# Retrieval from the memory in linear attention: one plain fp32 product against three split fp32r products, with feature map and memory each in a high and a low part

## The reference, cut to what matters

```python
B, H, S, D = 2, 8, 576, 64
scores = scale * q @ k.T ; causal mask ; a = softmax(scores)
local = a @ v
phi(x) = where(x > 0, x, exp(x) - 1) + 1
mem_ret = einsum('bhsd,bhde->bhse', phi(q), M_prev)          # the retrieval
mem_norm = einsum('bhsd,bhd->bhs', phi(q), z_prev) + 1e-6
out = g * mem_ret / mem_norm + (1 - g) * local               # g = sigmoid(beta), one per head
x = moe(out) ; result = moe2(x)
```

## Time and profile before

| | |
|---|---|
| median of 3 runs | 1149.52 us (1149.25 to 1149.59) |
| the profiled execution | 1149.53 us, its span 1147.7 us |
| TensorE busy | 1121.0 us (98%), 6932 matmuls |
| VectorE busy | 725.2 us (63%) |
| ScalarE busy | 513.6 us (45%) |
| GpSimd busy | 437.2 us (38%) |
| granted TensorE clock, mean | 0.997 of full speed |

### The profile page before, as it was taken

How to read it: one execution, slowest core, us unless ns; L and a number is a source line. 1 busy time by engine, 2 the same in 40 slices (tenths; PEclk the granted TensorE clock), 3 DMA queues, 4 the chain that set the end, 5 groups by cost and what they waited for, 6 DMA issues and landing times.

```text
span 1147.7 us, 21730 instructions
## 1 busy us (share of the span) xinstructions
PE 1121.0 (98%) x6932; PEld 1010.8 (88%) x6932; DVE 725.2 (63%) x1464; ACT 513.6 (45%) x1182; POOL 437.2 (38%) x506
## 2 busy tenths in 40 slices
PE   5999999999999999999999999999999999999998
PEld 3777779999999788898988989899999998998997
DVE  5888965345346877756566565675656656666564
ACT  4787867567567432443333333233332333323331
POOL 4778740000032442524425244352443433534331
PEclk8999999999999999999999999999999999999999
DMA  4513112002001101111111110111201111011002
GB/s 107 174 40 68 35 74 74 0 0 74 1 0 38 38 19 56 39 48 45 36 55 55 37 55 18 55 55 37 55 18 55 55 37 55 18 55 56 19 6 78
DMA packets 62128, 52.78 MB, mean 46 GB/s; under 512 B 32257, under 2 KB 49665, under 8 KB 62081
## 3 DMA queue, kind: packets, MB, share of 16 engines
q1 hardware_dynamic: 62080, 52.20, 14.9%
HBM read 49.83 MB, written 2.36 MB: 45 GB/s over the span
## 4 chain that ended last, share of the span: by engine, by line
PE 89%; DVE 4%; issue 3%; POOL 1%; ACT 1%; SPq 1%; DMA 0%; DVEq 0%; POOLq 0%; ACTq 0%
PE ps_y L1412 39%; PE ps_h L1412 26%; PE ps_g L1412 17%; PE ps_o L1412 2%; PE ps_s L1412 1%; PE ps_p L1441 1%; POOL prob L525 1%; PE ps_o L1453 1%; DVE zl L1181 1%; PE ps_y L1630 1%; DVE negmax L1031 0%; DMA beta_all<-in_beta_dram 0%; DVE nrm L1010 0%; DVE nrm_e L1014 0%; DVE ptl L974 0%
## 5 line engine op out<-in xcount | busy, mean ns | idle before, releaser
L832 ACT ACTIVATE zh<-h 128x256 fp32r<-128x256 f32 (+1 forms) x256 | 112.5, 445 | 332.5 <-POOL h L596 133.3
L1412 PE MATMUL ps_y<-w2c_h,zh 128*128 128x512 f32 x512 | 202.3, 395 | 0.2 <-DVE zl L1181 0.2
L1412 PE MATMUL ps_y<-w2c_l,zh 128*128 128x512 f32 x512 | 201.9, 394 | 0.0
L1412 PE MATMUL ps_y<-w2c_h,zl 128*128 128x512 f32 x512 | 199.3, 389 | 0.0
L591 POOL TENSOR_TENSOR h<-u,p 128x256 f32<-128x256 f32 (+1 forms) x64 | 57.0, 890 | 354.6 <-DVE u L1158 354.6
L1181 DVE SCALAR_TENSOR_TENSOR zl<-h,zh 128x256 fp32r<-128x256 f32 (+1 forms) x256 | 171.1, 673 | 7.2 <-ACT zh L832 6.6
L1412 PEld LDWEIGHTS ps_y<-w2c_h,zl 128*128 128x128 f32 x512 | 96.2, 188 | 21.9
L1412 PEld LDWEIGHTS ps_y<-w2c_h,zh 128*128 128x128 f32 x512 | 96.6, 189 | 13.9 <-DVE zl L1181 0.4
L1412 PEld LDWEIGHTS ps_y<-w2c_l,zh 128*128 128x128 f32 x512 | 96.6, 189 | 11.8
L1308 DVE SCALAR_TENSOR_TENSOR acc<-ps_y,weight,acc 128x512 f32<-128x512 f32 x112 | 82.1, 742 | 37.2 <-PE ps_y L1412 37.2
L596 POOL TENSOR_TENSOR h<-h,p 128x256 f32<-128x256 f32 (+1 forms) x64 | 61.0, 954 | 100.8 <-DVE h L1169 100.8
(11 more groups left out here) (212 smaller groups left out, 3086.2 us busy)
## 6 DMA issues: line engine op xcount, KB each, us to landing
rc<-in_moe_w_dram SPq DMA_DIRECT2D x64, 512.0 KB, 3.8
raw<-in_moe_w_in_dram SPq DMA_DIRECT2D x2, 2048.0 KB, 8.4
raw<-in_moe_w_out_dram SPq DMA_DIRECT2D x2, 2048.0 KB, 11.3
out_dram<-acc SPq DMA_DIRECT2D x9, 256.0 KB, 2.0
q_nat<-in_q_dram SPq DMA_DIRECT2D x16, 128.0 KB, 2.5
k_nat<-in_k_dram SPq DMA_DIRECT2D x16, 128.0 KB, 2.4
v_nat<-in_v_dram SPq DMA_DIRECT2D x16, 128.0 KB, 2.4
z_nat<-in_z_prev_dram SPq DMA_DIRECT2D x8, 64.0 KB, 3.0
```

The source lines that it names most:

```text
L832: act.activation(z_place(u, quarter, 0), rows, ACT.Relu).then_inc(e_hi, 1)
L1412: last = pe.matmul(dst, a[x], b[y], start=start and i == 0, stop=stop and i == 2)
```

## The change

The feature map of a pair is kept as `qph` and `qpl` and its memory as `mem_h` and `mem_l`, and the retrieval of each group becomes three split products. GpSimd makes `mem_l` at the start of the second part of `split_v`. VectorE makes `qpl` in `prep_lo`, now for items 3 and 4 too, in the loop at the steps `("item", 3)` and `("item", 4)`, and for pair 0 just ahead of the loop. ScalarE's copies go on as before, but release VectorE (`t_hi`) and no longer TensorE; `t_lo` is counted up by VectorE alone.

```diff
@@ -115,7 +115,8 @@
         vh, o = at_("vh", o, [P, 2, NJ, P], F32R)
         vl, o = at_("vl", o, [P, 2, NJ, P], F32R)
         mem_nat, o = at_("mem_nat", o, [P, P])
-        mem_t, o = at_("mem_t", o, [P, 2, P])
+        mem_h, o = at_("mem_h", o, [P, 2, P], F32R)
+        mem_l, o = at_("mem_l", o, [P, 2, P], F32R)
         z_nat, o = at_("z_nat", o, [P, P])
         phi_e, o = at_("phi_e", o, [P, NJ, P])
         phi_w, o = at_("phi_w", o, [P, NJ, P])
@@ -123,7 +124,8 @@
         qbl, o = at_("qbl", o, [P, 2, NQ, 2, QB], F32R)
         kh, o = at_("kh", o, [P, 2, S], F32R)
         kl, o = at_("kl", o, [P, 2, S], F32R)
-        qp, o = at_("qp", o, [P, 2, S])
+        qph, o = at_("qph", o, [P, 2, S], F32R)
+        qpl, o = at_("qpl", o, [P, 2, S], F32R)
         prob, o = at_("prob", o, [P, POFF[NQ]])
         pth, ptl = [], []
         for g in range(G):
@@ -386,7 +388,7 @@
                     sp.wait_ge(phi_exp, pair + 1)
                     sp.wait_ge(phi_relu, pair + 1)
                     load_heads(q_nat, q3, pair, ld_q)
-                    sp.wait_ge(v_split, 3 * pair + 3)
+                    sp.wait_ge(v_split, 4 * pair + 4)
                 else:
                     sp.wait_ge(nat_zeroed, 1)
                 load_heads(v_nat, v3, pair, ld_v)
@@ -448,7 +450,7 @@
         def _(pool):
             pool.sem_inc(phi_z, 1)
             pool.sem_inc(phi_q, 1)
-            pool.sem_inc(v_split, 3)
+            pool.sem_inc(v_split, 4)
             pool.sem_inc(s_eps, 9)
             pool.sem_inc(s_norm, 9)
 
@@ -504,10 +506,12 @@
                     settled()
                     pool.tensor_scalar(vh[:, half, :, :], v_nat[:, :, :], 1.0, 0.0, ALU.mult, ALU.add)\
                         .then_inc(v_split, 1)
-                    pool.tensor_scalar(mem_t[:, half, :], mem_nat[:, :], 1.0, 0.0, ALU.mult, ALU.add)\
+                    pool.tensor_scalar(mem_h[:, half, :], mem_nat[:, :], 1.0, 0.0, ALU.mult, ALU.add)\
                         .then_inc(v_split, 1)
                 else:
-                    pool.wait_ge(v_split, 3 * pair + 3 + 1)
+                    pool.wait_ge(v_split, 4 * pair + 4 + 2)
+                    pool.tensor_tensor(mem_l[:, half, :], mem_nat[:, :], mem_h[:, half, :].bitcast(F32),
+                                       ALU.subtract).then_inc(v_split, 1)
                     pool.tensor_tensor(vl[:, half, :, :], v_nat[:, :, :], vh[:, half, :, :].bitcast(F32),
                                        ALU.subtract).then_inc(v_split, 1)
 
@@ -631,7 +635,7 @@
         @block.scalar
         def _(act):
             act.preload_act_table_set("natural_log_exp_and_others")
-            act.sem_inc(t_hi, 3)
+            act.sem_inc(t_hi, 5)
             act.sem_inc(phi_exp, 1)
             act.sem_inc(phi_relu, 1)
             act.sem_inc(s_exp, 9)
@@ -658,10 +662,10 @@
                     last = copy(kh[:, half, NT * P:S], bank[:, P:P + TAIL])
                 elif item == 3:
                     act.wait_ge(o_ready, 3 * pair + 3)
-                    last = copy(qp[:, half, 0:NT * P], bank[:, :])
+                    last = copy(qph[:, half, 0:NT * P], bank[:, :])
                 else:
-                    last = copy(qp[:, half, NT * P:S], bank[:, 0:TAIL])
-                last.then_inc(t_hi if item < 3 else t_lo, 1)
+                    last = copy(qph[:, half, NT * P:S], bank[:, 0:TAIL])
+                last.then_inc(t_hi, 1)
 
             def phi(pair):
                 act.wait_ge(ld_q, 48 * pair + 48)
@@ -975,7 +979,7 @@
 
             def prep_lo(item, pair, half):
                 bank = prep_bank(item, pair)
-                dve.wait_ge(t_hi, 3 * pair + item + 4)
+                dve.wait_ge(t_hi, 5 * pair + item + 6)
                 rows_of = lambda h: slice(h * D, (h + 1) * D)
                 if item == 0:
                     for h in range(2):
@@ -985,6 +989,10 @@
                             scalar=SCALE, in1=qbh[r, half, 0:NQ - 1, h, :].bitcast(F32), op0=ALU.mult, op1=ALU.subtract)
                 elif item == 1:
                     last = less(kl[:, half, 0:NT * P], bank[:, :], kh[:, half, 0:NT * P])
+                elif item == 3:
+                    last = less(qpl[:, half, 0:NT * P], bank[:, :], qph[:, half, 0:NT * P])
+                elif item == 4:
+                    last = less(qpl[:, half, NT * P:S], bank[:, 0:TAIL], qph[:, half, NT * P:S])
                 else:
                     for h in range(2):
                         r = rows_of(h)
@@ -1065,7 +1073,7 @@
                     elif what == "x":
                         for group in group_at(t, pair, half, first):
                             x_lo(*group)
-                    elif what == "item" and more and t < 3:
+                    elif what == "item" and more:
                         prep_lo(t, pair + 1, 1 - half)
                     elif what == "phi" and more and t in (1, 3):
                         phi(t, pair + 1, 1 - half)
@@ -1092,6 +1100,8 @@
             row_sum(0, 0, 0)
             row_sum(1, 0, 0)
             dve.wait_ge(zeroed, 1)
+            for item in range(3, 5):
+                prep_lo(item, 0, 0)
             pairs(dve, body)
             probs_lo(NQ - 1, NP - 1, 1)
             x_lo(G - 2, NP - 1, 1)
@@ -1447,12 +1457,12 @@
 
                 pe.wait_ge(o_lo, 3 * pair + g + 3)
                 pe.wait_ge(t_lo, 5 * pair + 10)
-                pe.wait_ge(v_split, 3 * pair + 6)
+                pe.wait_ge(v_split, 4 * pair + 8)
                 cols = slice(3 * QB * g, 3 * QB * (g + 1))
 
-                pe.matmul(ps_o[:, 0:3 * P], mem_t[:, half, :],
-                          qp[:, half, cols].rearrange("p (b c) -> p b c", b=3).unsqueeze(2)
-                          .to_broadcast([P, 3, 2, QB]), start=True, stop=False)
+                products(ps_o[:, 0:3 * P], (mem_h[:, half, :], mem_l[:, half, :]),
+                         [x[:, half, cols].rearrange("p (b c) -> p b c", b=3).unsqueeze(2)
+                          .to_broadcast([P, 3, 2, QB]) for x in (qph, qpl)], True, False)
 
             def values(j, g, pair, half):
 
```

## The result

The changed kernel takes 1158.12 us (median of 6 runs, 1157.88 to 1158.84), the kernel before 1149.45 us on the same chip (6 runs, 1149.25 to 1149.84): a ratio of 1.0077 with an interval of 1.0064 to 1.009, so +8.7 us where +6.7 was forecast. It is slower, and the time lies within the range. The profiled execution took 1158.64 us (span 1156.7), 9.1 us more than the one of before; 0.4 us of this is not in the medians.

The account below looks back on a forecast made before the run. A ring of waits through the normalizer, with no engine full, was taken as the bound. 0.73 + 7 x (0.43 + 0.59 - 0.12) - 0.36 = +6.67 us gave 1156.2 us, range 1151.2 to 1160.

Parts of the forecast that it names:

- the range: Whole kernel: 1151.2 to 1160 us, the forecast's own part being 1154.5 to 1159.5.
- The bound and the sign: Attention loop: no engine is full, waits bound it; slower by over 0.2% was given 84%.
- the ring: Attention loop: waits closing once per 18.47 us period, two nearly equal legs, by TensorE and by ScalarE and GpSimd, through the normalizer.
- `mem_l`: GpSimd ahead of `vl`: 0.46 us long, delaying the normalizer through the end of `vl`; +0.43 us, 7 times.
- the sum: All terms: 0.73 + 7 x (0.43 + 0.59 - 0.12) - 0.36 = +6.67 us.
- The wait at item 4: TensorE's last feature-map transpose waits for VectorE's 512-column `qpl`, behind block 8's reciprocal: +0.59 us per pair.
- The retrieval: TensorE: three split products take 0.52 us against 0.65; 0.12 us less, counted once per pair in the loop.
- Block 8 behind the last `qpl`: TensorE's block 8 transposes wait for VectorE's last 64 columns; these just hide, by 0.06 us, so 0.
- Ahead of the loop: Pair 0's preparation: item 4 waits for VectorE's subtraction and the hop, +0.73 us once.
- The last three retrievals: After the last pair's preparation all three retrievals count: -0.36 us.
- TensorE itself carries the chain: After the last pair's preparation TensorE's own work was taken as the bound, so the last three retrievals count.

Follow-up runs that it names:

- e1: Kernel before with the retrieval as three fp32r products of the high parts alone, no low parts made; 1148.77 us, ratio 0.9996.
- e4: Changed kernel with GpSimd's `mem_l` moved behind `vl`; 1155.68 us, ratio 1.0054.
- e3: e1 plus the feature map's low part made by VectorE, which releases the banks; memory's low part left out; 1154.89 us, ratio 1.0046.
- e7: e4 with item 4's transpose behind the first value products of group 1 and block 8's transposes behind all of them; 1155.10 us, ratio 1.005.
- e6: Changed kernel with the moves of both e4 and e5; 1153.36 us, ratio 1.0036.
- e10: e7 plus the move of e5; 1155.41 us, ratio 1.005.
- e2: e1 plus the memory's low part made by GpSimd ahead of `vl`; feature map's low part left out; 1151.81 us, ratio 1.0022.
- e5: Changed kernel with VectorE's 512-column `qpl` of item 3 moved ahead of the reciprocal of block 8; 1155.69 us, ratio 1.0057.
- e9: Kernel before with only `vl` moved behind `prob` of block 8; 1152.08 us, ratio 1.0022.

## Why the prediction was right, and what was mis-sized

**The bound and the sign: right.** That a loss on either leg of the ring passes on whole is shown by the parts: 0.42 and 0.74 us a period by themselves, 1.15 together (18.43 in e1, 19.58 in the changed kernel, means of pairs 2 to 5).

**`mem_l`: right.** 0.46 us long as forecast, and 0.42 passes on against the 0.43 of the sum. e4 shows that it does so by the end of `vl`. The first pair pays as well, but by another way than the forecast's. There VectorE's normalizer is done ahead of `vl` (`nrm_g` at 32.41 + 0.17, `vl` at 32.51), and `phi_w` waits only for its turn in GpSimd's own queue: from the start of `vh` to that of `phi_w` it is 3.68 us (30.74, 34.42), 3.28 before (30.13, 33.41) and 3.28 in e3. So `mem_l` costs 0.40 there, and counting it seven times came out right.

**The wait at item 4: right in kind, 0.10 too small.** 0.59 was forecast; from the end of `prob` of block 7 to item 4 it is 0.69 longer. The subtraction started 0.20 us behind the reciprocal's start (97.26, 97.46), where I had taken 0.08; why, no run shows. Its 0.69 and the hop of 0.05 are as costed.

**The retrieval: a saving of the right size, by luck, that the wait ahead of it takes away.** I took 0.12 us off the period, from 0.65 for the plain product and 0.52 for the three. The three take 0.59 from start to start (98.40 to 98.99): the first takes 0.25 to the next start and not 0.17, in e7 too (95.19, 95.45), where nothing waits. e1 still saves 0.12 (0.81 against 0.93 us), of which the products are 0.60 against 0.65; the rest is the transpose ahead of them, 0.03 to the next start in e1 (92.34, 92.37) and 0.10 before. In the changed kernel that transpose stands behind a wait. From item 4 to the second value product is 0.97 us in the changed kernel and in e3, 0.16 more than in e1, where item 4 follows without a wait: the transpose takes 0.20 to the next start and not 0.03. So between item 4 and block 8 there is +0.06 and not -0.12 (fourth row of the table). **This, 0.18 us in each of seven periods, is the largest error of the sum.**

**Block 8 behind the last `qpl`: right that it hides**, and by more: `qpl` 128x64 ended at 99.20, TensorE came at 99.53. With the order of e7 it no longer hides.

**Ahead of the loop: 0.73 forecast, 0.61 measured**, by two errors of opposite sign, one of them the clock. The timeline, beside the earlier trace rows:

```profile
18.93 0.60 ACT L644 ACTIVATE qph<-ps_t 128x512 fp32r<-128x512 f32 x1 [1.85 <-issue]
19.63 0.69 DVE L978 TENSOR_TENSOR qpl<-ps_t,qph 128x512 fp32r<-128x512 f32 x1 [1.54 <-ACT qph L644]
...
20.38 0.47 PE L1416 MATMUL ps_t<-ident,phi_w 128*128 128x128 f32 x1 [1.53 <-DVE qpl L978]
```

Item 4 starts 0.83 later: I had left out the hop from ScalarE to VectorE, 0.10 us (19.53 to 19.63). Of this 0.22 came back by 24.66, where the score products of block 7 start (24.05 before), because TensorE's products became fast after less of the same work, as the last section says. That is luck of the execution: in e3 item 4 starts at 20.39, and the scores of block 7 only at 25.61, 1.56 later than before.

**The last three retrievals: -0.36 forecast, -0.04 measured**, from the first score product of the last pair's block 7 to the end of the span: 991.49 us before (1147.7 - 156.21), 991.45 after (1156.7 - 165.25), the spans being given to 0.1. The sentence that "TensorE itself carries the chain" there was wrong for the first two. The retrievals start 9.04 us later than before, as the scores of block 7 do (158.64 to 167.68, 162.30 to 171.34), the value products behind them only 8.92 and 8.91 later, so 0.12 to 0.13 is saved each time; but within the next two pieces of work the difference is 9.04 again (160.76 to 169.80, 164.03 to 173.07), since TensorE waits there. Behind the third it lasts for a while (172.49 to 181.39 is 8.90), and by the end of the span it is 9.00; where the rest went I did not follow.

**The sum again**, with the measured sizes: 0.61 + 7 x (0.42 + 0.69 + 0.06) - 0.04 = +8.8 us, against 8.7 between the medians. The seven periods' differences, pair 0 first, are 1.79, 0.84, 1.14, 1.15, 1.18, 1.12 and 1.21, together 8.43 where 7 x 1.17 gives 8.19. Pair 0 has the largest; a fall of the clock, as below, fits the 0.6 us that it has above the others. The close fit is in part luck, since this sum leaves out 0.13 us lost in the first row of the table already by e1 and the 0.15 gained in the fifth, which cancel.

**The range.** The parts that the prediction names for its own range, -0.9 and +0.4, +1.0, +1.4, reach from 1155.3 to 1159.0 us and not from 1154.5 to 1159.5. The measured time lies within both.

## What to carry to other kernels

A low part costs most where its making takes over the release of a buffer: look at what stands ahead of it on its engine as well as at its own length. Where a long GpSimd operation holds a small VectorE one that others wait for, put new GpSimd work behind the long one and not ahead of it. And a saving that stands just behind a new wait can be eaten by the start behind that wait (0.16 us here, against 0.12 saved), so cost the stretch from the wait on, not the products alone.

## What the hardware showed that I had not expected

**The clock fell once in the first pair.** Granted clock of TensorE in the changed kernel, columns as in the earlier trace rows:

```profile
34.00:36.00 2.00, 0.69 (x7) 0.56 (x7) 1.61 (x6) 0.00 (x0) 1.84 (x4) 1.00 1.05 390
36.00:38.00 2.00, 1.90 (x12) 1.32 (x10) 0.80 (x3) 1.51 (x5) 1.63 (x5) 0.82 1.18 314
38.00:40.00 2.00, 1.89 (x8) 1.60 (x7) 1.40 (x5) 1.31 (x5) 1.15 (x3) 0.50 0.88 155
40.00:42.00 2.00, 2.00 (x14) 1.90 (x13) 1.08 (x3) 1.07 (x5) 1.87 (x3) 0.83 0.66 150
```

It is at 0.50, the level of 1.2 GHz, in 38 to 40 us, after a stretch in which TensorE was busy for 0.69 of 2.00 us. In e6 and e10 it fell in the same stretch, after 0.66 of 2.00 us. That alone does not decide it: in e2 TensorE was busy for 0.67 us of 34 to 36 us, and the clock stayed at 1.00, as it did at 38 to 40 us in the kernel before, e3, e5 and e7 to e9. (e1 and e4 fell earlier, at 28 to 32 us.) The next pair's scores of block 7 start at 48.06; added up from e1 to e3 they would start at 47.46 (45.71 + 0.28 + 1.47), so an estimate of what the fall costs in this execution is 0.6 us; it is rough, as e1 has a fall of its own. It need not be in all executions: of the changed kernel's six, the two with a mean granted clock of 0.999 took 1158.64 and 1158.84 us, the four with 1.000 took 1157.88 to 1158.16. That these two are the ones with the fall fits, but only one of them was profiled.

**Products tell the clock better than its column.** Between 20.5 and 23.4 us the products of 384 columns start 0.32 us apart in the changed kernel although its clock column says 1.00, and 0.17 later on, at 2.4 GHz. In the kernel before the same products (21.29 to 21.61) have the same 0.32 us, and there the column says 0.50. The same stretch of work went over to the short distances at 23.3 us in the kernel before, between 23.4 and 23.7 in the changed one, between 24.5 and 25.2 in e4 and at 25.6 in e3. The Trainium skill (TensorE: Matmul & The Clock Gate, Part 1: The HAM clock gate) says that how long the slow level lasts at a kernel's start varies between runs of one kernel. The trace agrees, as far as kernels that run the same instructions on TensorE up to there can show it. It moved the start of block 7's scores from 24.66 (changed) to 25.61 us (e3).

**A hold has a sharp end.** The Trainium skill's lock (SBUF — State Buffer, Who interferes with whom) is for a whole instruction. The trace agrees and adds which: in e4 two GpSimd operations stand back to back, and `nrm_e` is let go with the first, 0.75 us long; in the changed kernel it starts in `vl` and is held to its end, 1.17 us.
